# Three products of a delta-rule triangular solve stream 32 instead of 64 columns per head

## What is computed

```python
for t in range(S):
    y[:, :, t] = einsum('bhd,bhde->bhe', q[:, :, t], state)
    v_old = einsum('bhde,bhd->bhe', state, k_n[:, :, t])
    state = state + beta[:, :, t] * einsum('bhd,bhe->bhde', k_n[:, :, t], v[:, :, t] - v_old)
```

## Time and profile before

| | |
|---|---|
| Median of 3 runs | 879.37 us (879.11 to 883.22) |
| The profiled execution | 885.98 us |
| Its span on the core | 884.0 us |
| TensorE busy | 808.4 us, 13,224 matmuls |
| DVE, ACT, POOL busy | 555.6, 434.6, 342.6 us |
| The attention, where the change is | about 22 to 384 us of the span |
| The dense blocks | about 384 us to the end |

### The profile page before, as it was taken

The page is one execution under the profiler, slowest core; times in us unless marked ns, Lnnn a source line. Parts: engine busy times, 40 slices in busy tenths (PEclk is TensorE's granted clock), DMA queues, the critical chain, the costliest instruction groups (busy, mean ns, idle before and its releaser), DMA issues. The chain is left out here.

```text
span 884.0 us, 30708 instructions
## 1 busy us (share of the span) xinstructions
PE 808.4 (91%) x13224; PEld 752.3 (85%) x13224; DVE 555.6 (63%) x1088; ACT 434.6 (49%) x833; POOL 342.6 (39%) x388
## 2 busy tenths in 40 slices
PE   1778988889888989899999999999999999999998
PEld 0667777778777777679999999999999999999998
DVE  3779887878787878748617436346365835646534
ACT  4747777676676767456224224234444433334221
POOL 4768787889787776405000000000012121121220
PEclk9989999999999999899999999999999999999999
DMA  7732222122222220310000000001400100100101
GB/s 250 228 133 69 69 67 73 58 76 65 72 71 70 63 58 14 119 37 21 1 1 1 1 0 0 0 1 63 171 36 1 54 1 1 54 0 0 54 1 53
DMA packets 26667, 46.56 MB, mean 53 GB/s; under 512 B 2736, under 2 KB 16560, under 8 KB 26544
## 3 DMA queue, kind: packets, MB, share of 16 engines
q1 hardware_dynamic: 26544, 44.74, 15.7%
HBM read 37.85 MB, written 4.72 MB: 48 GB/s over the span
## 5 line engine op out<-in xcount | busy, mean ns | idle before, releaser
L1359 POOL TENSOR_TENSOR vn_f<-vn_f 128x384 f32<-128x384 f32 x24 | 24.6, 1023 | 392.9 <-ACT vn_f L1404 392.9
L734 DVE TENSOR_TENSOR w_more<-t_ps,ident_band_lower 64x256 f16<-64x256 f32 x192 | 80.1, 417 | 12.5 <-PE t_ps L919 10.1
L521 ACT ACTIVATE t<-t_ps 128x512 f16<-128x512 f16 (+1 forms) x144 | 60.1, 417 | 39.9 <-PE t_ps L932 31.5
L1600 DVE TENSOR_TENSOR vn_pair<-vn_f,vn_pair 128x384 fp32r<-128x384 f32 x48 | 31.6, 661 | 58.8 <-ACT vn_pair L1366 58.8
L1157 PE MATMUL dense_ps<-w_spatial_pair,vn_pair 128*128 128x384 f32 x192 | 64.1, 334 | 0.0
L1158 PE MATMUL dense_ps<-w_spatial_pair,vn_pair 128*128 128x384 f32 x192 | 64.1, 334 | 0.0
L1159 PE MATMUL dense_ps<-w_spatial_pair,vn_pair 128*128 128x384 f32 x192 | 64.1, 334 | 0.0
L1536 DVE BATCH_NORM_STATS2 stats<-v_u_f 128x6 f32<-128x512 f32 x24 | 16.6, 694 | 63.2 <-ACT v_u_f L1424 63.1
L1157 PE MATMUL dense_ps<-w_in_pair,x_pair 128*128 128x512 f32 (+1 forms) x144 | 53.9, 374 | 0.0
L1775 PE MATMUL dense_ps<-w_spatial_pair,vn_pair 128*128 128x384 f32 x288 | 53.8, 334 | 0.0
L1366 ACT ACTIVATE g_pair<-v_u_f 128x384 fp32r<-128x384 f32 x32 | 16.8, 526 | 74.0 <-DVE v_u_f L1573 74.0
(11 more groups left out here) (233 smaller groups left out, 2584.0 us busy)
## 6 DMA issues: line engine op xcount, KB each, us to landing
qT_in<-in_q SPq DMA_DIRECT2D x24, 256.0 KB, 2.9
mask_beta<-in_beta_rows SPq DMA_DIRECT2D x48, 128.0 KB, 3.0
k_in<-in_k SPq DMA_DIRECT2D x24, 192.0 KB, 2.6
v_in<-in_v SPq DMA_DIRECT2D x24, 192.0 KB, 2.8
outT<-g_f SPq DMA_DIRECT2D x6, 576.0 KB, 3.1
w_spatial_f<-in_w_spT SPq DMA_DIRECT2D x3, 768.0 KB, 6.4
w_in_f<-in_k SPq DMA_DIRECT2D x3, 576.0 KB, 8.2
x_f<-in_k SPq DMA_DIRECT2D x3, 576.0 KB, 10.7
```

The lines of the kernel that those rows point to most:

```text
L521: return nc.scalar.activation(out, in_, ACT.Copy, scale=scale)
L734: tt(to, odd_even(whole_(ta[u % 2]), l)[r:r + C, :, :, 0, :], keep[r:r + C], ALU.mult).then_inc(w_ready[u % 2], 1)
L1359: tt(ta[:, r], ta[:, r], xt[:, r], ALU.mult).then_inc(zr_full, 1)
L1600: tt(zs[:, LO, r, n], a[:, r], zs[:, HI, r, n].bitcast(F32), ALU.subtract).then_inc(z_rest, 1)
```

## The change

The three products of a level read and write only the half of the columns that holds something or is read afterwards. L919 streams the even half of t into the even half of its bank, L932 the even half of w, and L941 the odd half of z into the odd half of its bank. `half_of` is a helper that was there before; it picks the runs of even (0) or odd (1) columns. Per head 32 columns are streamed, in runs of 2, 4, 8, 16 or 32 by level. No instruction is added, removed or moved: TensorE's list has the same 3,457 rows, and the weights of all three products are as before.

```diff
@@ level_w
             for h in range(H):
-                last = mm(ta[u % 2][:, h * C:h * C + C], nd[u % NS_][:, h, :], t[u % TS][:, h, :], start=True, stop=True)
+                last = mm(half_of(ta[u % 2][:, h * C:h * C + C], l, 0), nd[u % NS_][:, h, :], half_of(t[u % TS][:, h, :], l, 0),
+                          start=True, stop=True)
@@ level_t
                 for r in SIDES:
-                    last = mm(tile(ta[u % 2], r, h), z[u % ZS][r:r + C, h, :], w[l][r:r + C, h, r:r + C],
+                    last = mm(half_of(tile(ta[u % 2], r, h), l, 0), z[u % ZS][r:r + C, h, :], half_of(w[l][r:r + C, h, r:r + C], l, 0),
                               start=False, stop=True, skip_group_check=True)
@@ level_z
             for h in range(H):
-                last = mm(za[u % 2][:, h * C:h * C + C], w[l][:, h, :], z[u % ZS][:, h, :],
+                last = mm(half_of(za[u % 2][:, h * C:h * C + C], l, 1), w[l][:, h, :], half_of(z[u % ZS][:, h, :], l, 1),
                           start=l < NL - 1, stop=True, skip_group_check=True)
```

## The result

The changed kernel takes 893.33 us (median of 4 runs, 885.68 to 898.15) against 879.24 us before: a ratio of 1.0127, 95% interval 1.0079 to 1.0175. It is slower, by 11 us by the ratio and 14 by the medians. In a later set of runs it took 890.38 us (median of 4) against 879.02, 1.0107 (1.0062 to 1.0153). The granted clock tells the two kernels apart in every execution: its mean over an execution is 0.958 to 0.973 in all eight of the changed kernel, and 0.981 to 0.994 in the 88 of the kernel before that were run beside the experiments.

The account below looks back on a forecast made before the run. Instruction fetch, not TensorE's work, was taken to bound the steady part. Steady 0.9, start 0.1, 58 to 84 us 0.6 and end 0.4 sum to 2.0 us: 879.4 - 2.0 = 877.4 us, range 872.5 to 881.5.

Parts of the forecast that it names:

- The fetch: Steady part: blocks of some 256 instructions, 4.1 us each, set TensorE's pace and swallow most savings; chance 0.70, 877.4 us.
- TensorE's own savings: L919 and L941: 4.4 ns saved per matmul, 7.7 us at the full clock, 4.0 us at the slow one.
- the tile pairs: L932, 64 by 64 tiles in pairs: fewer columns buy nothing, 0 taken for the 1920 matmuls; other end 2 us.
- strides: Streaming halves in runs down to two elements instead of whole rows in the three products: cost taken as 0.
- The stops: TensorE running dry until the next instruction block comes; in the steady part they were to sum to 4 to 6 us more.
- the 20 places: Steady part: L966 waits for DVE's L743 in all 20 bodies, 6.7 us together; half of 1.8 us was given away.
- rival B: Whole kernel: the fetch is mostly hidden and TensorE's time is gained, 870.3 us, or 866 at 22 ns; chance 0.12.
- Rival C: Steady part: the granted clock falls where it has been full; 885.4 us from 4 more spells; chance 0.06.
- Some 2 us lost: Loss for each slow-clock spell of 6.8 us, a block's work becoming about 5.5 us against 4.1 us of fetch.
- The start: Before 84 us: 0.1 us gained ahead of 58 us and 0.6 us in 58 to 84 us.
- The 0.1 of 2.6 us: 13 groups before 51 us save 2.6 us, of which 0.1 comes through a wait for DVE in 53 to 58 us.
- the wait for L743: In 53 to 58 us TensorE waits 4.28 us for DVE; an earlier TensorE would only wait longer.

Follow-up runs that it names:

- strided64: The kernel before, with all three products streaming all 64 columns, sorted even runs first, with the change's strides: 880.87 us, ratio 1.0028.
- ident_whole: The kernel before, with each level's identity matmul streaming the whole 512 columns of t instead of the even half: 878.34 us, ratio 1.0002.
- first_four: The kernel before, with the change in all three products for units 0 to 3 of the 24 only: 885.0 us, ratio 1.0053.
- wz: The kernel before, with only products w and z streaming 32 columns, the correction of t keeping 64: 882.2 us, ratio 1.0043.
- t_only: The kernel before, with only the correction of t streaming 32 columns: 889.2 us, ratio 1.0124; run again, 885.1 us, ratio 1.0081.

## Why the prediction was wrong

**The fetch and TensorE's own savings: right.** w and z run at 26 ns by the 0.21 us of a group (25 was taken), the tile pairs keep their pace, strides show no price of note, and none of the saving comes through: 61.6 to 64.2 instructions for each us at the full clock with 32, 64 or, in the identity, twice the columns. From unit 9 to unit 15, where the kernel after is at the full clock throughout, it takes 82.4 us, strided64 83.3 and ident_whole, with the most to stream, 82.0. The stops are still there (21.1 us of idle time at t_ps in 84 to 366 us in the kernel after, 20.3 in the earlier trace rows). They were to grow by 4 to 6 us and didn't, since the slow spells leave next to none (16.88 of 17 us busy). Two slips in the prediction change nothing in this: the 20 places of the earlier trace rows are 8 of matmuls and 12 of weight loads, so not all 20 bodies wait there, and the lower end of rival B adds up to 865 us and not 866.

**Rival C is what happened, and it was given 0.06.** The step that failed stands in the prediction as "stops of up to 1.2 us have left it at 1.00 in all of 84 to 366 us". That row was read from a kernel that streams 64 columns between the stops, and it was used for one that doesn't. In the kernel after, five of the clock's seven falls behind its first rise came after stops no longer than those. These two rows stand just ahead of a fall, at 121 and 288 us:

```profile
120.24 0.34 PE L909 MATMUL t_ps<-ident_band_lower,z 64*64 64x64 f16 x10 [1.09 <-issue]
...
287.30 0.23 PE L933 MATMUL t_ps<-w_more,z 64*64 64x32 f16 x4 [1.11 <-issue]
```

Ahead of the falls at 131, 169 and 356 us the longest stops near by are 1.01, 0.77 and 0.34 us. The other two falls, at 322 and 380 us, follow longer ones, of 1.59 and 1.92 us, the second being the counterpart of the earlier trace rows; 34 of the 71.7 us of slow clock come behind these two. The fetch that hid the gain also made the danger: it gives TensorE a stop each 4 us, and with 64 columns streamed between such stops the clock stayed up (strided64, ident_whole, the kernel before), but for the one short spell of first_four. In w_only, which cuts w alone, it stayed up even behind stops of 1.40 and 1.31 us. With 32 columns in all three products it didn't. The forecast saw each of these and did not put them together.

**The price of a spell was about right, their number and length not.** "Some 2 us lost" was for 6.8 us. Measured it is a fifth of the spell (50.6 against 64.2 instructions for each us), 1.4 us for 6.8 and 3.6 for 17. But spells last up to 17 us here (6.8 before), and there are 71.7 us of them after the first rise, against 13.7.

**The start was mis-sized with the wrong sign.** It was to gain 0.6 us in 58 to 84 us; the prediction took the clock's first lasting rise, after 65 us, as given. The view's first record of a full clock is at 90 us in the kernel after (at 70 us in its second profile, with a spell from 77 to 87), and unit 3 is 6.0 us late. first_four shows that this is the first four units' own doing. The 0.1 of 2.6 us that was to come through before 58 us was not tested as it was meant, since TensorE came to the wait for L743 later and not earlier: at 55.23 us in place of 54.20. It waited 3.72 us in place of 4.28 and left it 0.5 us later, so the wait covered half of the delay.

**The sum, put right.** 97 us more at the slow clock (39 ahead of the first rise, 58 behind it) by a fifth is 19 us if TensorE were the bound all through; 12.0 are lost by unit 23. The likely reasons are the start, where waits for DVE cover part of the slower work, and the profiled execution of before, which was slow at the full clock too (61.6 instructions for each us in its steady part, where strided64 and ident_whole have 62.6 and 62.3 with the fall at the end counted in). Beside those two profiles (875.22 and 877.56 us) the profiled 898.15 us are 21 to 23 us more, so the fifth is about the right size.

**What stays open.** Whether and why the tiles of t weigh more than w and z together, though they use a quarter of the array: the ratios point to it (1.0124 and 1.0081 against 1.0043), with intervals that overlap, and no run says why. Why the steady part keeps its clock with any one product cut and loses it with all three: no run has two of them cut with t among them. And the 0.4% of w alone, whose profile has no more slow time than that of the kernel before. The 0.2% of z alone, if it is one, would fit the clock: its first record of a full clock is at 69 us and unit 3 passes at 102.1 us; but wz, with z cut too, passes unit 3 at 98.6.

## What to carry to other kernels

Before streaming less on an engine that stops and starts, look at what the clock did between the stops: work that is hidden behind a fetch or a wait may be what keeps it up, and taking that away can cost more than its own time is worth. When TensorE stops at even distances with no semaphore behind it, count instructions between the stops; if the count is constant (some 255 here), cutting columns can gain nothing, as here, where cutting 768 instructions gained 8 us. And a margin read from the kernel before ("stops of this length did no harm") holds only for what the change leaves alone.

## What was not expected of the hardware

TensorE at 1.2 GHz showed itself *busier* (16.88 of 17 us) than at 2.4 GHz (89%), and stayed slow for up to 17 us in that state, so a high busy share beside a low clock was no sign that it was about to rise. The mean clock that goes with a profile is a weak guide as well: a slow stretch before its first record isn't in it, and in t_only it read 0.985 and 0.988 with a loss of about 1%.
